# Attention and mixture of experts on one core: the order of the turns in attention, passes of 64 instead of 128 tokens, and a third path

## The chip, the cores and the metric

The kernel runs on one core of one Trainium2 chip. A core has TensorE (matrix products), VectorE, ScalarE and GpSimd (POOL) for the rest, and SyncE, which here only issues DMA transfers. The metric is the device time of one execution in microseconds; the median of three executions is 398.88 us (398.73 to 399.06).

## What is computed

Windowed attention with 8 heads over 4 batches of 576 tokens, then each token goes to one of 8 experts (two layers, ReLU between), and its row is scaled by its gate value:

```python
scores = scale * np.matmul(q, k.transpose(0, 1, 3, 2))
bias = slopes[:, None, None] * (-np.abs(rel).astype(np.float32))[None, :, :]
mask = (rel >= 0) & (rel < window)                    # window = 128
scores = np.where(mask, scores + bias[None], -1000000000.0)
attn = softmax(scores); x = attn @ v                  # x: 2304 rows of 512
logits = x @ w_gate; expert_idx = np.argmax(logits, axis=1)
h = np.maximum(x_e @ w1[e], 0.0)                      # per expert, 512 -> 1024
y = h @ w2[e]; out[i] = gate_w[i] * y                 # 1024 -> 512
```

With the inputs of the reference the eight experts get 373, 244, 350, 293, 183, 193, 328 and 340 tokens. The capacity of 576 drops none.

## The kernel before

**Attention.** Queries are taken in 18 tiles of 128 tokens, in two spans of 9, and each tile in two steps of four heads ("quads"): 18 steps (`kk`) in each of two calls of `batch`. In one step TensorE does, in the order written in `batch` of the tensor block: a turn (four transposes) of the q rows (even steps) or k rows (odd steps) of the tile two ahead into the one PSUM bank `turn_ps`; the transposes of this step's probabilities (`turn_probs`); the turn back of the mix of the step before, with the gate logits (`turn_back`); the scores of the step two ahead (`score`); and the mix of this step (`mix`), first with `v_rows`, then with `v_step`, the difference of two tiles' v. ScalarE copies the mix (`copy_mix`), the turned q (`turned_q`) and the turned probabilities (`turned_probs`), and takes the exponentials of the next step (`exps`). VectorE copies the turned k, replaces masked scores (`pick`), adds the bias and takes minima (`bias_minimum`), and scales the result (`normalise`). GpSimd masks the turned probabilities (`keep_later`, line 624), makes `v_step` (line 605) and, in steps 4 to 19, splits the first expert's weights into a high and a low part (lines 616 and 617). A bank is shared by the scores of a step and the turn back of the step before the last, so `turn_back` waits for `biased`, the minima of the scores that lay there. The routing of the tokens (top expert, ranks, slots) is put between these steps in the second call: `early_counts` at `kk` 4 and 13, a first inversion at `kk` 10, and at `kk` 14 the turn of a first gathered tile of expert 0, whose low part VectorE makes at line 1036.

**Experts.** Every product is three matmuls, of high and low parts. Expert 0's first tile has code of its own (`first_...`). Then follow eight groups, `group(n)`: for `c` in 0 to 9, `step` runs chunk `c` of the first layer (12 matmuls, up to `c` = 7, with the tokens as the moving columns) and chunk `c - 2` of the second layer (3 matmuls of 512 columns for each tile of 128 tokens). One pass is one `c`. Group 0 has two tiles. The others have three where the expert has more than 256 tokens, and else two: a branch on a register (`third`, lines 1512 and 1514) picks one of two blocks of code in each pass. The register is loaded at line 1580 in front of each group. ScalarE takes the ReLU's high part of each chunk (`relu`), VectorE the low part (`lower`), and both split the next expert's weights (`split_hi`, `split_lo`), a piece per chunk. The rows of the next group are gathered by GpSimd and turned by TensorE behind passes 3, 4 and 5 (`turn_rows`, tiles 0 to 2; tiles 0 and 2 use the same PSUM bank). All three tiles are turned, used or not. At the group's end `weigh_all` scales each output tile on VectorE and GpSimd scatters it to `out` (line 694); in the last pass the three tiles end one behind the other. `make_tables` computes on VectorE, in group 0 behind `lower` of chunk 0, what the scatter and some rest tiles need.

## Time and profile before

| | |
|---|---|
| median of three executions | 398.88 us |
| the profiled execution | 398.74 us, span 397.0 us |
| mean granted clock of TensorE | 0.993 |
| TensorE busy | 378.6 us, 95% of the span |
| VectorE, ScalarE, GpSimd busy | 252.9, 202.7, 144.4 us |
| attention | up to about 135 us |
| first tile, routing | about 135 to 153 us |
| eight groups | about 153 to 386 us |
| scatter and end | 386 to 397 us |

Times inside the trace are microseconds from the start of the span. A matmul's length in a row is that of its way through the array, and the next one starts before it ends. So what a matmul costs is the distance from one start to the next. Idle time of an engine counts only where somebody waits for it.

### The profile page before, as it was taken

The numbers are of one execution on the slowest core, as the hardware profiler recorded it, in microseconds if no ns is written. First come the engines' busy times: TensorE is split into PE (matmuls) and PEld (weight loads), VectorE is DVE, ScalarE is ACT, GpSimd is POOL, SyncE is SP. The second block draws the span as 40 slices with busy tenths as digits, with TensorE's granted clock in tenths as the row PEclk, the third lists the DMA queues.
The fourth block names the chain that finished last, engine by engine and source line by source line (L and its number), as shares of the span: only waits on it lengthen the run. The fifth ranks groups of instructions, "written<-read, shape, count | busy, mean of one in ns | idle before, by whom it ended". The sixth has DMA issues, their size and how long they took to land.

```text
span 397.0 us, 8382 instructions
## 1 busy us (share of the span) xinstructions
PE 378.6 (95%) x2990; PEld 327.4 (82%) x2990; DVE 252.9 (64%) x796; ACT 202.7 (51%) x535; POOL 144.4 (36%) x192
## 2 busy tenths in 40 slices
PE   7899999998999999999999999999999999999990
PEld 7688777887877778889998989899999899999970
DVE  6787787799898555967665545556768674441120
ACT  2978788886877425536634415434646444411100
POOL 7549989835743432042250121024051340020002
PEclk9999999999999999999999999999999999999997
DMA  9998999999720121887666356354777673010001
GB/s 167 205 305 208 236 225 233 272 260 211 151 85 34 49 45 52 270 260 245 195 226 201 114 181 223 115 187 147 234 254 227 201 223 132 2 54 17 2 2 70
DMA packets 81314, 64.71 MB, mean 163 GB/s; under 512 B 63982, under 2 KB 63982, under 8 KB 81264
## 3 DMA queue, kind: packets, MB, share of 16 engines
q1 hardware_dynamic: 73600, 52.19, 48.2%
q0 software_dynamic: 3840, 11.03, 8.6%
q10 hardware_dynamic: 3824, 0.80, 1.2%
q8 instruction: 34, 0.56, 0.6%
q14 instruction: 16, 0.13, 0.1%
HBM read 54.56 MB, written 11.02 MB: 165 GB/s over the span
## 4 chain that ended last, share of the span: by engine, by line
PE 76%; POOL 10%; DVE 6%; issue 2%; DMA 2%; ACT 1%; SPq 1%; POOLq 0%; DVEq 0%
PE ps L1472 57%; PE ps L1330 4%; POOL weights_sb L617 4%; PE ps L1303 4%; PE ps L1341 3%; PE ps L1465 3%; PE ps L1269 2%; DMA q_rows<-in_q 2%; POOL probsT L624 2%; PE ps L1311 2%; POOL v_step L605 2%; POOL weights_sb L616 2%; DVE ps L905 1%; DVE probs L918 1%; POOL out L694 1%
## 5 line engine op out<-in xcount | busy, mean ns | idle before, releaser
L1472 PE MATMUL ps<-rowsT_hi,weights_sb 128*128 128x256 f32 (+1 forms) x512 | 120.7, 313 | 0.7 <-DVE rowsT_lo L1156 0.7
L1472 PE MATMUL ps<-weights_sb,hiddenT 128*128 128x512 f32 x480 | 118.3, 392 | 0.8 <-DVE hiddenT L1173 0.8
L1472 PEld LDWEIGHTS ps<-weights_sb,hiddenT 128*128 128x128 f32 x480 | 88.1, 188 | 17.3 <-DVE hiddenT L1173 1.0
L855 ACT ACTIVATE hiddenT<-ps 128x384 fp32r<-128x384 f32 (+1 forms) x64 | 30.6, 479 | 117.3 <-PE ps L1472 110.7
L1472 PEld LDWEIGHTS ps<-rowsT_hi,weights_sb 128*128 128x128 f32 x512 | 87.6, 188 | 2.2 <-DVE rowsT_lo L1156 1.1
L1181 DVE TENSOR_TENSOR weights_sb<-raw,weights_sb 128x1024 fp32r<-128x1024 f32 x56 | 68.5, 1223 | 18.1 <-ACT weights_sb L843 15.2
L1472 PE MATMUL ps<-rowsT_lo,weights_sb 128*128 128x256 f32 (+1 forms) x256 | 79.0, 309 | 0.0
L1173 DVE SCALAR_TENSOR_TENSOR hiddenT<-ps,hiddenT 128x384 fp32r<-128x384 f32 (+1 forms) x64 | 34.5, 539 | 62.1 <-ACT hiddenT L855 62.1
L843 ACT ACTIVATE weights_sb<-raw 128x1024 fp32r<-128x1024 f32 x56 | 58.9, 1052 | 0.2 <-DMA raw<-in_moe_w 0.2
L680 POOL DMA_INDIRECT gathered<-x_rows,src_row x21 | 21.7, 1035 | 95.5 <-DVE weight_now L1167 90.9
L694 POOL DMA_INDIRECT out<-y_sb,dst_row x21 | 24.4, 1161 | 86.9 <-DVE y_sb L1187 82.6
L741 ACT ACTIVATE probs<-probs,mins 128x128 f32<-128x128 f32 x144 | 55.6, 393 | 0.4 <-DVE mins L918 0.4
L1472 PEld LDWEIGHTS ps<-rowsT_lo,weights_sb 128*128 128x128 f32 x256 | 48.2, 188 | 1.1
L624 POOL TENSOR_SCALAR_AFFINE_SELECT probsT<-probsT 128x512 f32<-128x512 f32 x32 | 20.4, 638 | 41.6 <-ACT probsT L767 41.6
L1303 PE MATMUL ps<-kT,qT 64*64 64x192 f32 (+3 forms) x480 | 28.8, 332 | 0.0
L741 ACT ACTIVATION_READ_ACCUMULATOR probs<-probs,mins 128x1 f32 x144 | 27.7, 192 | 0.0
L767 ACT ACTIVATE probsT<-ps 128x512 f32<-128x512 f32 x36 | 21.4, 594 | 10.2 <-PE ps L1311 10.2
L1341 PE MATMUL ps<-eye_wg,mixT 128*128 128x144 f32 x144 | 24.2, 291 | 2.5 <-DVE mins L918 2.5
L905 DVE COPY_PREDICATED ps<-later,ps 128x256 f32<-128x256 int32 (+1 forms) x64 | 22.1, 391 | 4.9 <-PE ps L1303 4.7
L947 DVE TENSOR_TENSOR x_sb<-ps,inv_sums 128x256 f32<-128x256 f32 x36 | 15.3, 424 | 15.3 <-PE ps L1341 13.5
L1187 DVE TENSOR_SCALAR y_sb<-ps,weight_now 128x512 f32<-128x512 f32 x23 | 15.9, 745 | 14.2 <-PE ps L1472 14.2
L1330 PE MATMUL ps<-probsT,v_rows 128*64 128x128 f32 x288 | 23.7, 285 | 0.1
(173 smaller groups left out, 494.2 us busy)
## 6 DMA issues: line engine op xcount, KB each, us to landing
raw<-in_moe_w SPq DMA_DIRECT2D x64, 512.0 KB, 4.4
q_rows<-in_q SPq DMA_DIRECT2D x16, 256.0 KB, 5.9
v_rows<-in_v SPq DMA_DIRECT2D x16, 256.0 KB, 5.2
x_rows<-x_sb SPq DMA_DIRECT2D x16, 256.0 KB, 4.5
k_rows<-in_k SPq DMA_DIRECT2D x14, 256.0 KB, 6.3
k_rows<-in_k ACTq DMA_DIRECT2D x2, 256.0 KB, 6.7
v_rows<-in_v SPq DMA_DIRECT2D x4, 128.0 KB, 5.9
v_front<-in_v SPq DMA_DIRECT2D x4, 128.0 KB, 6.4
```

Of the source, the lines that this page charges most:

```text
L624: g.affine_select(out=probsT[:, 1, :, :], in_=probsT[:, 0, :, :], compare_op=ALU.is_gt, fill=0.0, base=0, pattern=[[0, QUAD], [-1, P]], ch ...
L694: g.indirect_dma_start(out, bass.IndirectOffsetOnAxis(ap=rows[:, i:i + 1], axis=0), y_sb[:, i, :], None, bounds_check=N - 1, oob_is_err=Fa ...
L741: last = nc.scalar.activation(pr, pr, ACT.Exp, bias=mins[:, kk % 2, n:n + 1], scale=-1.0, accum_out=sums[:, i, h:h + 1])
L843: nc.scalar.activation(weights_sb[:, parity(e), 2 * layer, RAW * j:RAW * (j + 1)], raw[:, j, :], ACT.Copy).then_inc(w_hi[layer], 1)
L855: nc.scalar.activation(hiddenT[0][c % RINGED][:, 0:P * size], hiddenT_ps(c, size), ACT.Relu).then_inc(hiddenT_hi, 1)
L905: vec.copy_predicated(both[:, :, 2 * P - earlier[i]:2 * P], later[:, own].bitcast(I32).unsqueeze(1).broadcast_to([P, 2, earlier[i]]), both ...
L1173: vec.scalar_tensor_tensor(out=hiddenT[1][c % RINGED][:, 0:P * size], in0=hiddenT_ps(c, size), scalar=0.0, in1=hiddenT[0][c % RINGED][:, 0 ...
L1181: vec.tensor_tensor(weights_sb[:, parity(e), 2 * layer + 1, part], raw[:, j, :], weights_sb[:, parity(e), 2 * layer, part].bitcast(F32), A ...
L1303: ins = te.matmul(scores_ps(kk % 2, odd)[rows, 2 * P * n + first:2 * P * n + last], qT[part, u % 2, h // 2, rows], keys, start=True, stop= ...
L1330: last = te.matmul(mixT_ps[DH * odd:DH * odd + DH, n, :], left[:, DH * h:DH * h + DH], probsT[:, part, 2 * odd + n, :], start=(part == 0), ...
L1341: last = te.matmul(back_ps(kk % 2)[:, c, :], mixT[:, c, :], eye_wg[:, 2 * quad + c, :], start=True, stop=True)
L1472: ins = te.matmul(dst, left[a], right[c], start=first and n == 0, stop=last and n == 2)
```

## The change

In attention the turn of q or k goes behind the transposes of the probabilities (except in the very first step), and ScalarE copies the turned q behind the exponentials. The routing's counts and the first inversion go ahead of `turn_back`. VectorE makes the first tile's low part behind the minima of its step. In the expert layers, tile 1 of group 0 is turned right behind tile 0. `third` has three values: none, half (up to 320 tokens, first-layer passes of 320 columns instead of 384) and whole. A third tile that isn't used isn't turned. The register for the next group is loaded at the start of a group. `make_tables` is cut in two, and its long part goes to group 1. In the last group the last three chunks of the second layer run tile by tile.

```diff
@@ ScalarE, batch
+                    if first and kk == 0:
+                        turned_q(b, 2)
+                    turned_probs(b, kk)
+                    if not (last and kk == STEPS - 1):
+                        exps(b + (kk + 1) // STEPS, (kk + 1) % STEPS)
-                    if quad == 0 and not (last and i + 2 >= TI):
+                    if quad == 0 and not (last and i + 2 >= TI) and not (first and kk == 0):
                         turned_q(b + (i + 2) // TI, (i + 2) % TI)
...
-                    turned_probs(b, kk)
-                    if not (last and kk == STEPS - 1):
-                        exps(b + (kk + 1) // STEPS, (kk + 1) % STEPS)
@@ VectorE
-            vec.tensor_scalar(third_i[:, :], tiles_of[:, :], float(SIDE), None, ALU.is_ge).then_inc(sizes_ready, 1)
+            counts = late_ranks_ps[:, E * FULL:E * FULL + E]
+            link(vec.tensor_scalar(extra[:, :], counts, float(P * (SIDE - 1)), None, ALU.is_gt))
+            vec.scalar_tensor_tensor(out=third_i[:, :], in0=counts, scalar=float(P * (SIDE - 1) + HALF),
+                                     in1=extra[:, :], op0=ALU.is_gt, op1=ALU.add).then_inc(sizes_ready, 1)
...
-                    if n == 0 and c == 0:
+                    if n == 0 and c == 2:
+                        make_targets()
+                    if n == 1 and c == 2:
                         make_tables()
@@ TensorE, batch
-                    if turns and quad == 0:
...
+                    if first and kk == 0:
+                        turn_next()
+                    turn_probs(b, kk, 0)
+                    turn_probs(b, kk, 1)
+                    if not (first and kk == 0):
+                        turn_next()
...
-                    turn_probs(b, kk, 0)
-                    turn_probs(b, kk, 1)
-                    if first and kk == 1:
-                        pe.wait_ge(wg_landed, 48)
-                    if not (first and kk == 0):
-                        turn_back(b + (kk - 1) // STEPS, (kk - 1) % STEPS)
                     if last and kk == FIRST_INVERTED:
...
+                    if not (first and kk == 0):
+                        turn_back(b + (kk - 1) // STEPS, (kk - 1) % STEPS)
@@ TensorE, experts
+            def last_chunks(n, size):
+                for i in range(size):
+                    for c in range(FC - RINGED, FC):
+                        if i == 0:
+                            pe.wait_ge(hiddenT_ready, n * FC + c + 1)
+                        last = product(y_ps(i), [part[c % RINGED][:, P * i:P * i + P] for part in hiddenT],
+                                       [weights(parity(n), kind, D * c, D) for kind in (2, 3)], False, c == FC - 1)
+                    last.then_inc(y_done[i], 1)
...
+            def turn_third(n, third):
+                with pe.If(third > 0):
+                    turn_rows(n, SIDE - 1)
+                with pe.If(third < 1):
+                    pe.wait_ge(rowsT_ready, tile_count(n, 0))
+                    pe.sem_inc(rows_turned[SIDE - 1], 1)
...
             def group(n, third):
+                after = third_of(n + 1) if n + 1 < E else None
                 for c in range(FC + RINGED - 1):
...
-                        with pe.If(third > 0):
+                        with pe.If(third > 1):
                             step(n, SIDE, c)
+                        with pe.If(third < 2):
+                            with pe.If(third > 0):
+                                step(n, SIDE, c, HALF)
                         with pe.If(third < 1):
                             step(n, SIDE - 1, c)
...
             turn_rows(0, 0)
-            first_second_layer(range(FC - 2, FC - 1))
             pe.wait_ge(filled_ready, 1)
             turn_rows(0, 1)
-            first_second_layer(range(FC - 1, FC)).then_inc(first_y_done, 1)
+            first_second_layer(range(FC - 2, FC)).then_inc(first_y_done, 1)
             rows_and_weights(0)
-            group(0, None)
+            pe.wait_ge(sizes_ready, 1)
+            third = group(0, None)
```

The order of TensorE in an odd step of attention (step 1; `probs` are the probabilities, `k_rows` the turn, `mixT` the turn back), before:

```order
L1269 MATMUL ps<-ident,k_rows 128x128 [waits k_landed2,qT_ready]
L1269 MATMUL ps<-ident,k_rows 128x128 x3
L1311 MATMUL ps<-ident,probs 128x128 [waits probs_ready]
L1311 MATMUL ps<-ident,probs 128x128
L1311 MATMUL ps<-ident,probs 128x128 [waits probs_ready]
L1311 MATMUL ps<-ident,probs 128x128
L1341 MATMUL ps<-eye_wg,mixT 128x144 [waits mixT_ready,biased,wg_landed]
```

and after:

```order
L1324 MATMUL ps<-ident,probs 128x128 [waits probs_ready]
L1324 MATMUL ps<-ident,probs 128x128
L1324 MATMUL ps<-ident,probs 128x128 [waits probs_ready]
L1324 MATMUL ps<-ident,probs 128x128
L1282 MATMUL ps<-ident,k_rows 128x128 [waits k_landed2,qT_ready]
L1282 MATMUL ps<-ident,k_rows 128x128 x3
L1354 MATMUL ps<-eye_wg,mixT 128x144 [waits mixT_ready,biased,wg_landed]
```

The two kinds of transposes have changed places; what each waits for is the same.

TensorE from the turn of group 0's first tile (`gathered`) to the first matmul of group 0 (`rowsT_hi`), before:

```order
L1465 MATMUL ps<-ident,gathered 128x128 [waits gather_done0]
L1465 MATMUL ps<-ident,gathered 128x128 x3
L1472 MATMUL ps<-weights_sb,first_hiddenT_hi 128x512 x2
L1472 MATMUL ps<-weights_sb,first_hiddenT_lo 128x512
L1465 MATMUL ps<-ident,gathered 128x128 [waits gather_done1,filled_ready]
L1465 MATMUL ps<-ident,gathered 128x128 x3
L1472 MATMUL ps<-weights_sb,first_hiddenT_hi 128x512 x2
L1472 MATMUL ps<-weights_sb,first_hiddenT_lo 128x512
L1472 MATMUL ps<-rowsT_hi,weights_sb 128x256 [waits w1_split,rowsT_ready]
```

and after:

```order
L1486 MATMUL ps<-ident,gathered 128x128 [waits gather_done1,filled_ready]
L1486 MATMUL ps<-ident,gathered 128x128 x3
L1493 MATMUL ps<-weights_sb,first_hiddenT_hi 128x512 x2
L1493 MATMUL ps<-weights_sb,first_hiddenT_lo 128x512
L1493 MATMUL ps<-weights_sb,first_hiddenT_hi 128x512 x2
L1493 MATMUL ps<-weights_sb,first_hiddenT_lo 128x512
L1550 TENSOR_LOAD third_i [waits sizes_ready,w1_split,rowsT_ready]
L1550 ISA x2
L1493 MATMUL ps<-rowsT_hi,weights_sb 128x256
```

The second turn stands three matmuls earlier, and the load of the register now stands behind the wait for the turned rows and ahead of the first matmul.

## Rows read from the trace of the kernel before

**Rows 1.** Waits of TensorE, whole run: us in total, times, longest.
```profile
PE ps L1341 <- DVE mins L918: 2.5, 3, 1.1
...
PE ps L1472 <- DVE hiddenT L1173: 0.8, 1, 0.8
PE ps L1472 <- DVE rowsT_lo L1156: 0.7, 1, 0.7
```
**Rows 2.** Timeline, attention: start us, length us, engine, line; in brackets idle, releaser.
```profile
31.46 0.33 PE L1269 MATMUL ps<-ident,q_rows 128*128 128x128 f32 x1
...
48.77 1.28 POOL L617 TENSOR_TENSOR weights_sb<-raw,weights_sb 128x512 fp32r<-128x512 f32 x1
...
50.66 0.64 POOL L624 TENSOR_SCALAR_AFFINE_SELECT probsT<-probsT 128x512 f32<-128x512 f32 x1 [0.61 <-ACT probsT L767]
...
69.61 0.33 PE L1269 MATMUL ps<-ident,k_rows 128*128 128x128 f32 x1
...
78.62 0.33 PE L1269 MATMUL ps<-ident,q_rows 128*128 128x128 f32 x1
...
81.97 0.33 PE L1269 MATMUL ps<-ident,k_rows 128*128 128x128 f32 x1
```
**Rows 3.** Timeline, attention: first steps, counts of the routing, first tile's low part.
```profile
15.07 0.20 PEld L1311 LDWEIGHTS ps<-ident,probs 128*128 128x128 f32 x2 [0.20 <-ACT probs L741]
...
86.94 0.20 PE L1352 MATMUL ps<-onehot,below 128*128 128x72 bf16 x1
...
87.58 0.72 PE L1303 MATMUL ps<-kT,qT 64*64 64x192 f32 x12
...
125.04 0.69 DVE L1036 TENSOR_TENSOR first_rowsT_lo<-ps,first_rowsT_hi 128x512 fp32r<-128x512 f32 x1
```
**Rows 4.** Timeline of TensorE in the expert layers, passes of 256 and 384 tokens.
```profile
172.29 0.28 PE L1472 MATMUL ps<-rowsT_lo,weights_sb 128*128 128x256 f32 x1
...
173.59 0.63 PE L1472 MATMUL ps<-weights_sb,hiddenT 128*128 128x512 f32 x2
...
214.84 0.51 PE L1472 MATMUL ps<-rowsT_hi,weights_sb 128*128 128x384 f32 x2
...
216.57 2.25 PE L1472 MATMUL ps<-weights_sb,hiddenT 128*128 128x512 f32 x9
...
218.66 0.60 PE L1465 MATMUL ps<-ident,gathered 128*128 128x128 f32 x4
...
219.28 0.34 PE L1472 MATMUL ps<-rowsT_lo,weights_sb 128*128 128x384 f32 x1
```
**Rows 5.** Timeline of VectorE before expert 0's group, and line 1580: ns, first and last start.
```profile
151.00 0.69 DVE L1156 TENSOR_TENSOR rowsT_lo<-ps,rowsT_hi 128x512 fp32r<-128x512 f32 x1 [2.81 <-ACT rowsT_hi L848]
...
152.13 0.69 DVE L1156 TENSOR_TENSOR rowsT_lo<-ps,rowsT_hi 128x512 fp32r<-128x512 f32 x1 [0.43 <-ACT rowsT_hi L848]
...
L1580 PEldq TENSOR_LOAD <-third_i x7: 301/312/483, 174.8 to 349.1; - x7
...
L1580 PEldq SEQ_ASSERT  x7: 18/18/28, 175.6 to 349.8; - x7
```
**Rows 6.** Timeline of VectorE in group 0, and line 1514 as in rows 5.
```profile
155.35 0.30 DVE L1218 SCALAR_TENSOR_TENSOR is_free<-is_free,src_f 128x144 f32<-128x144 f32 x1
...
159.31 0.17 DVE L1241 TENSOR_SCALAR column_i<-column_f 128x18 int32<-128x18 f32 x1
...
L1514 PEldq COMPARE_BRANCH  x70: 72/210/353, 176.2 to 382.1; - x70
```
**Rows 7.** DMA queues of the page: packets, MB, share of 16 engines.
```profile
q8 instruction: 34, 0.56, 0.6%
```
**Rows 8.** Timeline of the end.
```profile
385.18 2.07 DVE L1187 TENSOR_SCALAR y_sb<-ps,weight_now 128x512 f32<-128x512 f32 x3 [3.87 <-PE ps L1472]
386.72 0.98 POOL L694 DMA_INDIRECT out<-y_sb,dst_row  x1 [29.80 <-DVE y_sb L1187]
...
389.30 0.99 POOL L694 DMA_INDIRECT out<-y_sb,dst_row  x1 [0.30 <-issue]
```

More of the change, by code:

```diff
@@ L337, in attention_moe @@
         is_full_ready = sem("is_full_ready")
-        rows_turned = sem("rows_turned")
+        rows_turned = [sem(f"rows_turned{i}") for i in range(SIDE)]
         rowsT_hi = sem("rowsT_hi")
@@ L669, in gather @@
                 if not (isinstance(n, int) and n == 0):
-                    pool.wait_ge(rows_turned, tiles_before(n))
+                    for i in range(sides(n)):
+                        if not (isinstance(n, int) and n == 1 and i == SIDE - 1):
+                            pool.wait_ge(rows_turned[i], n if i < SIDE - 1 else n - 1)
                     pool.wait_ge(weight_kept, n)
@@ L1057, in batch @@
                             bias_minimum(b + (kk + 2) // STEPS, (kk + 2) % STEPS, odd)
+                    if last and kk == STEPS - 4:
+                        dve.wait_ge(first_rows_hi, 1)
+                        vec.tensor_tensor(first_rowsT[1][:, :, :], turn_ps.rearrange("p (c s) -> p c s", c=DC),
+                                          first_rowsT[0][:, :, :].bitcast(F32), ALU.subtract
+                                          ).then_inc(first_rows_ready, 1)
                     if last and since == 1:
@@ L1220, in make_tables @@
                 vec.tensor_copy(dst_row[:, :], is_free[:, :]).then_inc(dst_ready, 1)
+            def make_tables():
                 te = [P, TABLE, E]
@@ L1428, in batch @@
                         n = 0 if kk == 4 else 1
+                        pe.wait_ge(mixT_ready, b * STEPS + kk)
                         pe.wait_ge(onehot_ready, n + 1)
                         early_counts(n).then_inc(ranked, 1)
+                    if first and kk == 1:
+                        pe.wait_ge(wg_landed, 48)
+                    if not (first and kk == 0):
+                        turn_back(b + (kk - 1) // STEPS, (kk - 1) % STEPS)
                     if not (last and kk + 2 >= STEPS):
@@ L1476, in weights, with first_layer @@
                 return weights_sb[:, slot, kind, at:at + size]
-            def first_layer(n, size, c):
+            def first_layer(n, tokens, c):
                 for d in range(DC):
-                    last = product(hiddenT_ps(c, size), [weights(parity(n), kind, F * d + P * c, P) for kind in (0, 1)],
-                                   [part[:, d, 0:P * size] for part in rowsT[parity(n)]], d == 0, d == DC - 1)
+                    last = product(hiddenT_ps(c, tokens), [weights(parity(n), kind, F * d + P * c, P) for kind in (0, 1)],
+                                   [part[:, d, 0:tokens] for part in rowsT[parity(n)]], d == 0, d == DC - 1)
                 last.then_inc(hidden_done, 1)
@@ L1494, in second_layer, with step @@
                         last.then_inc(y_done[i], 1)
-            def step(n, size, c):
-                if c < FC:
-                    first_layer(n, size, c)
-                if c >= RINGED - 1:
+            def last_chunks(n, size):
[6 more added lines that the diff above has]
+                    last.then_inc(y_done[i], 1)
+            def step(n, size, c, spared=0):
+                if c < FC:
+                    first_layer(n, P * size - spared, c)
+                by_tiles = isinstance(n, int) and n == E - 1
+                if by_tiles and c == FC + RINGED - 2:
+                    last_chunks(n, size)
+                elif RINGED - 1 <= c < (FC - 1 if by_tiles else FC + RINGED - 1):
                     second_layer(n, size, c - (RINGED - 1))
@@ L1517, in group @@
                                 pe.sem_inc(y_done[SIDE - 1], 1)
-                    if c in TURNED_AT and n + 1 < E:
+                    if c in TURNED_AT[:-1] and n + 1 < E:
                         turn_rows(n + 1, c - TURNED_AT[0])
+                    if c == TURNED_AT[-1] and n + 1 < E:
+                        turn_third(n + 1, after)
+                return after
             def first_tile_chunks(half, chunks):
```

39 lines of the change are left out of this document (19 added, 20 removed).

## Prediction

> **What bounds the kernel now.** I read the waits of TensorE first. TensorE is busy 95% of the span, and of the little that it waits, three pieces lie behind the start: 2.5 us in three waits of the turn back for VectorE's minima, 0.8 us in group 0 for the low part of a hidden chunk, and 0.7 us in front of group 0 for the low part of the turned rows [rows 1]. All else must be sought in the distances between its starts. In attention an undisturbed step of TensorE lasts 3.35 us (from the turn at 78.62 to that at 81.97), but the eleven steps from 31.46 to 69.61 last 38.15 us and not 36.85 [rows 2]. GpSimd splits weights there, and the rows show why it holds the others up though it isn't full: its subtraction ends at 48.77 + 1.28 = 50.05, then it sits idle for 0.61 us until ScalarE has copied the turned probabilities, and masks them at 50.66 [rows 2]. In the groups TensorE runs without a gap but one, and everything else has slack. So the expert part gets shorter only by less work on TensorE, by closing those two waits, or by a shorter tail behind its last matmul.
>
> **The sum is made against the profiled execution's 398.74 us,** 0.14 below the median. The 1.74 us outside the span stay.
>
> **Attention, GpSimd's stretch: -1.3.** The turn no longer stands ahead of the probabilities. A turn of four transposes costs about 0.45 us (from 218.66 to 219.28 is one turn and one matmul of 0.173, below) [rows 4]. So ScalarE's copy and GpSimd's mask can start about 0.45 us earlier in the step. GpSimd's work in a pair of steps is the pair's length less the idle 0.61, and the pair lasts about 2 x 38.15 / 11 = 6.94: that is 6.3 us, less than TensorE's 2 x 3.35 = 6.70. TensorE becomes the bound, and the excess of 38.15 - 36.85 = 1.3 goes. The bounds are 0 (something else holds the steps at their length) and -1.5. The q that ScalarE now copies last is wanted by the next step's k turn, which itself stands later; I give that nothing. It would cost at most what ScalarE lacks in one step, and it has idle time in every step there.
>
> **Attention, first steps: +0.3.** In step 1 the exponentials aren't ready: TensorE turned k and still waited 0.20 us for them, until 15.07 [rows 3]. With the turn behind, it has nothing to fill with, and the whole turn of 0.45 to 0.5 comes after. What was hidden is now in the open, less the time for which the first half of the probabilities can go ahead. Bounds 0 and 0.5.
>
> **Attention, counts ahead of the turn back: +0.65.** The 14 small matmuls of the counts last 87.58 - 86.94 = 0.64 us [rows 3]. They stood behind `turn_back`, where they held up only the scores. Now they hold up the turn back too, and behind it VectorE's `normalise`, which stands ahead of the next `pick`. It is from these three places (`kk` 4, 10 and 13) that VectorE's long stretches start at whose ends TensorE waits the 2.5 us [rows 1]. VectorE has some slack before each, so not all of 0.64 arrives. I take 0.25, 0.3 and 0.1. Bounds 0 and 1.6 (three times the 0.64, less one smaller group).
>
> **Attention, low part of the first tile: -0.6.** Its 0.69 us at 125.04 [rows 3] stood in VectorE's queue ahead of the minima for which TensorE waits at the third place, one of the three waits of [rows 1]. Behind them it is wanted only ten microseconds later. The minima come 0.69 earlier less the 0.1 above, and that wait is about as long. Bounds 0 and -0.7. Attention in all: -0.95.
>
> **In front of group 0: +0.2.** Here two edits pull against each other. With tile 1 turned right behind tile 0, ScalarE and VectorE can run back to back: the first low part lasts from 151.00 to 151.69, and the second can then end at about 152.3 instead of 152.13 + 0.69 = 152.82 [rows 5], if the gathered rows have landed by then. That alone would take 0.5 of the 0.7 us wait. But the register's load now stands behind that very wait and ahead of the first matmul, where TensorE's queue is empty. A load and what belongs to it takes from 174.8 to 175.6 in its first instance, and 0.7 in its last [rows 5]. Between the groups this is hidden, because the sequencer runs ahead of the array: the trace has no gap at 174.8. Here it has nothing to hide behind. -0.5 + 0.7 = +0.2. Bounds -0.5 (hidden after all) and +0.4.
>
> **The hole in group 0: -0.8.** `make_tables` holds VectorE from 155.35 to 159.48 [rows 6], and the low part of chunk 1 comes 0.8 us too late for TensorE [rows 1]. The short part that stays (two of the operations) stands behind chunk 2, when that chunk is done. The long part, about 3.3 us, goes to group 1 behind chunk 2. Who waits there is the low part of chunk 3, which TensorE wants two passes later, and two passes of a two-tile group last 2 x 2.8 us (12 x 0.118 + 6 x 0.232, both below). VectorE has the split of one piece (1.2) to do besides, so about 1 us of slack remains. Bounds -0.9 and 0.
>
> **Turns of unused third tiles: -1.2.** Experts 1, 4 and 5 have 256 tokens or fewer. Three turns at 0.36 to 0.45 [rows 4], all on a TensorE that doesn't wait. ScalarE and VectorE still copy.
>
> **Half passes: -2.65.** Only expert 3, with 293 tokens, is between 257 and 320. The distance between matmuls of 256 columns is (173.59 - 172.29) / 11 = 0.118 us, with 384 it is (216.57 - 214.84) / 10 = 0.173 [rows 4]. A straight line gives 0.0275 less for 320 than for 384, times 8 x 12 = 96 matmuls: 2.65 us. The second layer has the tokens as weights and doesn't change. Its distance of 0.232 ((218.66 - 216.57) / 9) stays [rows 4]. Nothing near the 0.118 of the narrower pass can stop a distance of 0.146, so both loading and streaming allow it. Bounds -2.65 and 0.
>
> **More branches: 0.** In each of the 70 passes one more comparison, or two, is executed. One that jumps took 0.21 us, one that falls through 0.07 [rows 6]. So the sequencer needs some 0.3 us more for each pass, and a pass lasts at least 1.4. The cover is the sequencer's lead, which hid 0.7 to 0.8 us of loading between groups.
>
> **The end: -1.25.** Output tiles used to end 3 matmuls apart, now they end 9 apart (2.1 us). The last one ends when it did, and VectorE's scaling with it, at 385.18 + 2.07 = 387.25. But the scatters were queued on GpSimd: the first started at 386.72, 0.8 after its tile's scaling, and the third only at 389.30 [rows 8]. Now the two before it are long gone, and it starts at 387.25 + 0.8 = 388.05. 1.25 earlier; what follows it is the same. The wait for the last hidden chunk has only 6 matmuls of cover (1.4 us) instead of 18; the ReLU and low part take about that, so I give 0 and at worst 0.2.
>
> **Sum:** -0.95 + 0.2 - 0.8 - 1.2 - 2.65 - 1.25 = -6.65, so 392.1 us.
>
> **Rivals.** *VectorE or ScalarE takes GpSimd's place in attention.* The steps keep their length, or the three stretches of VectorE grow by all of 0.64 each. For it speaks that VectorE's stretches start from places that come later now; against it, that between 30 and 80 us VectorE has idle time in each step. It gives 0 to +1.5 for attention instead of -0.95: 393.0 to 394.5, say 393.6.
>
> *The half passes don't pay, or aren't taken* (the distance stays at 0.173, or the register says 2 for expert 3). Nothing in the trace has 320 columns. 392.1 + 2.65 = 394.7.
>
> *More goes than I count* (the load hidden, the counts harmless): 392.1 - 0.7 - 0.65 = 390.7.
>
> *Code loading makes it slower.* Each pass now holds three blocks of code. By the order of instructions a group of the seven has 492 matmuls instead of 324, each with its load of weights, so the program grows by 7 x 168 x 2 = 2,350 instructions, from about 9,200. The 34 packets of the instruction queue carried 0.56 MB [rows 7]: the growth is some 9 packets more. A packet took 0.006 x 16 x 397 / 34 = 1.1 us. If each is in the open, TensorE stands for 9 x 1.1 = 10 us, and the time is 402; it decides from 0.75 us for each. Against it: the 34 of now leave no gap in the groups. Advanced Engine Details and Errata (ISA Cache) in the Trainium skill says that a line of the instruction cache holds 16 KB or 256 instructions, which agrees with 0.56 MB in 34 packets.
>
> **How the numbers follow.** 0.64 for my sum, 0.2 for the steps of attention that don't gain, 0.06 for the half passes that don't pay, 0.06 for more, 0.04 for code loading. The range of 390.4 to 394.7 takes in the first four. A measurement of this kernel can tell about 0.2% (0.8 us) from no change. All cases but the last lie clearly below 398.1: faster 0.95, same 0.01, slower 0.04.
>
> **What would show it.** Turns 3.35 us apart between 31 and 70 us. A wait of the turn back after the counts that has grown at the first two places and nearly gone at the third. No wait for hiddenT in group 0, and a gap of about 0.9 us in front of group 0 with the register's load in it. 96 matmuls of 320 columns in one group, 0.145 apart, and 80 transposes of gathered rows instead of 92. The last scatter about 1.3 us closer to TensorE's last matmul. I am wrong if TensorE shows gaps at the passes' starts, if the low part of chunk 3 of group 1 is waited for, or if attention ends no earlier.

## Result: 1.0% faster, and attention longer instead of shorter

| | before | changed |
|---|---|---|
| median | 398.97 us (398.73 to 399.41, 4 runs) | 395.06 us (393.71 to 395.72, 4 runs) |
| the profiled execution | 398.74 us, span 397.0 | 393.71 us, span 391.9 |
| mean granted clock in the profile | 0.993 | 0.994 |

The ratio is 0.990 (95% interval 0.988 to 0.992). The direction was right and the size wrong: 392.1 was forecast, and the median lies 0.4 us above the range. Two things need an explanation: the profiled execution is 1.6 us slower than the sum, and it is the fastest of four, whose times spread over 2.0 us.

I cut the trace where the first tile's first matmul starts, where group 0 starts, and at the last matmul's start:

| stretch, us | before | changed | difference | forecast |
|---|---|---|---|---|
| up to the first tile (attention) | 135.58 | 136.45 | +0.87 | -0.95 |
| first tile, to the start of group 0 | 17.30 | 17.58 | +0.3 | +0.2 |
| eight groups, to the last matmul's start | 233.13 | 228.16 | -4.97 | -4.65 |
| from there to the end of the span | 11.02 | 9.71 | -1.31 | -1.25 |

So the expert part did what the sum said, and attention alone failed, by 1.8 us. The arrival of the first q and k differs from run to run: the first mix starts at 13.32 instead of 13.64 here, so counted from there attention grew by 1.2. I number attention's steps from 0 to 35 (the second span begins with 18) and measure each from the start of the last mix of the step before to that of its own.

| step | before | changed | what is new |
|---|---|---|---|
| 1 | 3.31 | 3.58 | the turn is in the open |
| 6 to 15, each | 3.40 to 3.52 | 3.35 | GpSimd no longer holds them up |
| 16 | 3.51 | 3.19 | the same |
| 20 | 3.40 | 4.21 | the turn back waits 0.54 |
| 22 | 4.09 | 4.38 | counts ahead of the turn back |
| 24 | 4.80 | 5.36 | the turn back waits 1.29 instead of 1.11 |
| 28 | 3.67 | 3.97 | inversion ahead of the turn back |
| 30 | 4.29 | 4.04 | |
| 31 | 3.98 | 4.23 | counts ahead of the turn back |
| 33 | 3.86 | 3.65 | the low part no longer in the way |
| 34 | 2.68 | 3.35 | the turn back waits 0.98 |

GpSimd's stretch gained what it should. In the timeline of TensorE, eleven steps after the probabilities' transposes at 31.41 come those at 68.11: 36.70 us, against 38.15 between the turns of [rows 2].

```profile
31.41 0.66 PE L1324 MATMUL ps<-ident,probs 128*128 128x128 f32 x4
...
68.11 0.66 PE L1324 MATMUL ps<-ident,probs 128*128 128x128 f32 x4
```

The waits of TensorE, changed kernel (us in total, times, longest), answer to [rows 1]. The turn back waits longer and oftener, the wait for `hiddenT` in group 0 is gone, and small ones are new, two of them of the mix. The counts and the inversion write to a bank that the mix uses too, and VectorE reads them only behind `normalise`, which waits for the turn back. Before, the counts stood between the turn back and the mix and gave VectorE that time. Now they stand ahead of both, and the mix waits.

```profile
PE ps L1354 <- DVE mins L922: 3.7, 5, 1.3
...
PE ps L1493 <- DVE rowsT_lo L1163: 1.0, 1, 1.0
...
PE ps L1343 <- DVE own_rank L996: 0.3, 1, 0.3
PE ps L1343 <- DVE first_slot L1049: 0.2, 1, 0.2
```

**What the minima waited for.** I looked at what GpSimd (POOL) and VectorE (DVE) do ahead of the three long waits, at steps 20, 24 and 34. The columns are start, length, engine, line, and in brackets the idle time with its releaser.

```profile
75.81 1.27 POOL L617 TENSOR_TENSOR weights_sb<-raw,weights_sb 128x512 fp32r<-128x512 f32 x1
75.96 1.15 DVE L938 TENSOR_TENSOR sums_eps<-sums,eps 128x8 f32<-128x8 f32 x1
78.77 0.51 PE L1354 MATMUL ps<-eye_wg,mixT 128*128 128x144 f32 x2 [0.54 <-DVE mins L922]
...
90.38 0.63 POOL L624 TENSOR_SCALAR_AFFINE_SELECT probsT<-probsT 128x512 f32<-128x512 f32 x1 [3.74 <-ACT probsT L769]
90.40 0.64 DVE L1015 TENSOR_SCALAR past<-rounded 128x9 f32<-128x9 f32 x1
90.98 1.28 POOL L605 TENSOR_TENSOR v_step<-v_rows 128x512 f32<-128x512 f32 x1
91.08 1.21 DVE L1016 SCALAR_TENSOR_TENSOR key<-best,past 128x9 f32<-128x9 f32 x1
95.21 0.76 PE L1354 MATMUL ps<-eye_wg,mixT 128*128 128x144 f32 x4 [1.29 <-DVE mins L922]
...
128.13 0.69 DVE L1059 TENSOR_TENSOR first_rowsT_lo<-ps,first_rowsT_hi 128x512 fp32r<-128x512 f32 x1
...
128.69 1.27 POOL L605 TENSOR_TENSOR v_step<-v_rows 128x512 f32<-128x512 f32 x1
128.80 1.22 DVE L1025 TENSOR_SCALAR in_tile<-iota_p,within,mark 128x128 f16<-128x128 f16 x1
...
132.01 0.76 PE L1354 MATMUL ps<-eye_wg,mixT 128*128 128x144 f32 x4 [0.98 <-DVE mins L922]
```

An addition of 8 numbers in each row lasts 1.15 us. Each of these VectorE operations starts just behind one of GpSimd's, and ends 0.03 to 0.06 us behind it: 77.11 and 77.08, 91.04 and 91.01, 92.29 and 92.26, 130.02 and 129.96. Where no GpSimd operation runs beside them in the same trace, they last 0.16, 0.17, 0.16 and 0.31 us. The kernel before has two of these places too, but there it is a shorter GpSimd operation that they meet. At step 1, where it meets a `v_step`, the addition lasts 1.13 us even there:

```profile
15.54 1.13 DVE L934 TENSOR_TENSOR sums_eps<-sums,eps 128x8 f32<-128x8 f32 x1
...
77.10 0.58 DVE L934 TENSOR_TENSOR sums_eps<-sums,eps 128x8 f32<-128x8 f32 x1
...
91.27 0.59 DVE L1012 SCALAR_TENSOR_TENSOR key<-best,past 128x9 f32<-128x9 f32 x1
```

The Trainium skill, SBUF — State Buffer, SBUF: two separate sides, says that VectorE and GpSimd share a pair of ports, which the one that starts first holds for its whole instruction while the other is fully blocked. By the same section VectorE needs the pair in a mode that takes both ports, or with two SBUF inputs while GpSimd's instruction reads SBUF. The trace agrees: `sums_eps` and `key`, with two SBUF inputs, are held, and `x_sb`, which reads one operand from PSUM, lasts 424 to 426 ns in all its 36 instances, among them twelve that lie wholly within a GpSimd subtraction. `past` and `in_tile` have one SBUF input and are held too. In which mode they run, no trace shows.

**The expert part.** In front of group 0 TensorE waits 1.01 us instead of the 0.71 that the kernel before shows as 0.7 in [rows 1]. The low part of the rows was ready by 151.86 + 1.29 = 153.15. The register's load, of which the first row gives the first and last start behind the lengths in ns, and what belongs to it are over only at 153.9.

```profile
L1550 PEldq TENSOR_LOAD <-third_i x7: 301/308/484, 153.2 to 312.0; - x7
...
L1550 PEldq SEQ_ASSERT  x7: 18/18/28, 153.9 to 312.5; - x7
```

The timeline of VectorE and TensorE there:

```profile
151.86 1.29 DVE L1163 TENSOR_TENSOR rowsT_lo<-ps,rowsT_hi 128x512 fp32r<-128x512 f32 x2 [2.82 <-ACT rowsT_hi L852]
...
152.62 0.40 PE L1493 MATMUL ps<-weights_sb,first_hiddenT_lo 128*128 128x512 f32 x1
154.03 0.38 PE L1493 MATMUL ps<-rowsT_hi,weights_sb 128*128 128x256 f32 x1 [1.01 <-DVE rowsT_lo L1163]
```

In the groups, by shape (count | busy us, mean ns): 96 matmuls of 320 columns, and 80 transposes instead of 92.

```profile
L1493 PE MATMUL ps<-rowsT_hi,weights_sb 128*128 128x320 f32 x64 | 15.3, 312 | 0.0
L1486 PE MATMUL ps<-ident,gathered 128*128 128x128 f32 x80 | 11.8, 272 | 0.0
L1493 PE MATMUL ps<-rowsT_lo,weights_sb 128*128 128x320 f32 x32 | 9.9, 310 | 0.0
```

In TensorE's timeline six distances between starts lie from 247.58 to 248.46, 0.147 us each. A straight line had given 0.1455.

```profile
247.58 0.31 PE L1493 MATMUL ps<-rowsT_lo,weights_sb 128*128 128x320 f32 x1
...
248.46 0.31 PE L1493 MATMUL ps<-rowsT_lo,weights_sb 128*128 128x320 f32 x1
```

Split at the turns' starts, the -4.97 is -1.07 up to the first turn in group 0 (the hole), -1.36 for the three unused tiles and -2.62 for expert 3's group; under 0.1 is left. The queue of instructions, on the page, answers to [rows 7]: ten packets more, and no start in the groups is over 0.1 us late.

```profile
q8 instruction: 44, 0.72, 0.8%
```

At the end the last scatter is issued at 384.16, 1.97 us after the last matmul's start. In [rows 8] it is issued at 389.30, 3.29 us after.

```profile
380.10 0.98 POOL L696 DMA_INDIRECT out<-y_sb,dst_row  x1 [27.09 <-DVE y_sb L1196]
382.09 0.98 POOL L696 DMA_INDIRECT out<-y_sb,dst_row  x1 [1.00 <-DVE y_sb L1196]
384.16 0.98 POOL L696 DMA_INDIRECT out<-y_sb,dst_row  x1 [1.09 <-DVE y_sb L1196]
```

### The profile page after: what moved, and what is told of

Its sections match the earlier page's. It is cut to its first block, busy times and chain, and to the rows that moved or that the text cites. A ratio compares the mean times of both kernels' runs of the same rounds, so it can differ in the third digit from the quotient of the medians.

```text
span 391.9 us, 8491 instructions
## 1 busy us (share of the span) xinstructions
PE 373.1 (95%) x2978; PEld 323.0 (82%) x2978; DVE 253.9 (65%) x797; ACT 202.3 (52%) x535; POOL 144.6 (37%) x192
## 3 DMA queue, kind: packets, MB, share of 16 engines
HBM read 54.56 MB, written 11.02 MB: 167 GB/s over the span
## 4 chain that ended last, share of the span: by engine, by line
PE 86%; DVE 7%; DMA 2%; ACT 1%; issue 1%; SPq 1%; POOL 0%; DVEq 0%; POOLq 0%
PE ps L1493 59%; PE ps L1343 7%; PE ps L1316 5%; PE ps L1354 4%; PE ps L1324 4%; PE ps L1282 3%; PE ps L1486 2%; DMA q_rows<-in_q 2%; DVE ps L909 1%; DVE probs L922 1%; DVE x_sb L951 1%; DVE kT L932 1%; PE ps L1400 0%; SPq L444 0%; PE ps L1360 0%
## 5 line engine op out<-in xcount | busy, mean ns | idle before, releaser
L1493 PE MATMUL ps<-rowsT_hi,weights_sb 128*128 128x256 f32 (+2 forms) x512 | 118.2, 309 | 1.0 <-DVE rowsT_lo L1163 1.0
L1493 PE MATMUL ps<-rowsT_lo,weights_sb 128*128 128x256 f32 (+2 forms) x256 | 78.2, 306 | 0.0
L1324 PE MATMUL ps<-ident,probs 128*128 128x128 f32 x144 | 23.8, 287 | 0.3 <-ACT probs L743 0.3
```

Source lines behind the costliest of these rows:

```text
L1324: last = te.transpose(probsT_ps[:, P * (2 * odd + n):P * (2 * odd + n) + P], probs[:, kk % 2, 2 * odd + n, :], ident[:, :])
L1493: ins = te.matmul(dst, left[a], right[c], start=first and n == 0, stop=last and n == 2)
```

## Experiments

Two theories stood against each other for attention. H1: VectorE's short operations meet GpSimd's long ones at other places now, and are held for longer. H2: counts and inversion ahead of the turn back cost all of it. The kernel before had medians of 398.96, 398.93, 399.26 and 398.98 us beside the four sets of runs.

**The changed kernel again, and the old order of attention**

> The changed kernel once more, nothing edited. Its first four times ran from 393.71 to 395.72 us, and the lowest goes with the highest mean granted clock (0.994 against 0.990). Theory S (the spread is TensorE's clock falling once or twice behind an idle stretch, most likely the 1.0 us in front of group 0): the times fall again between 393.5 and 396, with the mean clock, and a profile of a slower one shows a slice at 1.2 GHz that the first profile doesn't have. Rival: nothing but the chip's DMA differs: the times spread without the clock.

Measured: 394.87 us median (393.66 to 396.85, 6 runs), ratio 0.990 (0.987 to 0.993). The times spread as forecast, but not for the reason forecast. The mean clock is between 0.987 and 0.994 and follows the time only in part: the slowest run, 396.85, has the lowest, but the fastest, 393.66, has 0.991, and one of 395.21, the profiled one, has 0.993. In that profile step 20 lasts 3.40 us: GpSimd waited 0.84 us for rows of v ahead of it, so its subtraction began only at 77.27, behind the addition at 76.54. Step 24 lasts 5.34, and step 28 5.19 instead of 3.97:

```profile
111.29 0.42 DVE L951 TENSOR_TENSOR x_sb<-ps,inv_sums 128x256 f32<-128x256 f32 x1 [2.52 <-PE ps L1354]
...
112.24 0.66 PE L1343 MATMUL ps<-probsT,v_rows 128*64 128x128 f32 x8 [1.45 <-DVE first_slot L1049]
```

The profile models the turn back named in the first row to end by 109.97, but its signal stands in the trace at 111.20, 1.2 us later. In the first profile it came 0.02 us behind the modelled end. It is this signal that `x_sb` waited for. `normalise` waits for stored rows (`rows_stored`) only ahead of a tile's first quad, and this is the second. Behind `x_sb` stand `first_slot` and the mix, so a whole step moves. Why the signal came late isn't shown.

> The changed kernel with the order of attention of the kernel before (ScalarE's batch, the first tile's low part on VectorE, the turn ahead of the probabilities, counts and inversion behind the turn back), everything else as changed. The traces put first matmul of the first tile at 135.58 us before and 136.45 after. Theory A (attention's reordering lost 0.9 us net, all the gain is in the experts): 0.9 less than the changed kernel, ratio to it 0.998, and against before -5.9 us. Rival B (the prediction's own step, attention gains 0.95): 0.9 more than the changed kernel. If the granted clock also falls less often here, more than 0.9.

```diff
-                    turn_probs(b, kk, 0)
-                    turn_probs(b, kk, 1)
-                    if not (first and kk == 0):
-                        turn_next()
+                    if turns and quad == 0:
+                        if not (first and kk == 0):
+                            pe.wait_ge(kT_ready, tb * TI + ti)
+                        turn_q(tb, ti)
+                    if turns and quad == 1:
+                        pe.wait_ge(qT_ready, tb * TI + ti + 1)
+                        turn_k(tb, ti)
...
+                    turn_probs(b, kk, 0)
+                    turn_probs(b, kk, 1)
+                    if first and kk == 1:
+                        pe.wait_ge(wg_landed, 48)
+                    if not (first and kk == 0):
+                        turn_back(b + (kk - 1) // STEPS, (kk - 1) % STEPS)
                     if last and kk == FIRST_INVERTED:
...
```

ScalarE's and VectorE's batches are put back too. Measured: 393.56 us (393.14 to 393.93, 5 runs), ratio 0.986 (0.984 to 0.988). It is 1.3 us faster than the changed kernel on the same chip, and its times spread over 0.8 us instead of 3.2. Theory A holds by the medians. The trace of this run doesn't show the loss: attention ends at 136.38, 0.07 ahead of the changed kernel's. There too a signal came late: that of the scores stands at 111.29, 1.4 us behind their modelled end, and steps 29 and 30 last 4.14 and 4.66 us instead of the 3.35 and 4.29 of the kernel before.

**GpSimd waits**

> The changed kernel in which GpSimd waits, in the second span alone, with three of its instructions until VectorE is past its short operations (sums_eps; the keys): the split's last subtraction, the mask of step 5 of that span, and each v_step. Nothing is left out. Theory H1 (steps 20, 24 and 34 are long since VectorE's short SBUF operation is held for as long as a GpSimd tensor-tensor of 1.28 us runs): sums_eps at step 19 lasts 0.15 to 0.6 and not 1.15, key at step 24 0.17 and not 1.21, past 0.17 and not 0.64, in_tile at step 33 0.31 and not 1.22; the waits of the turn back, 0.54, 1.29 and 0.98 us, shrink to nothing, 0.1 and 0.1, and attention ends 2.0 to 2.6 us earlier. Theory H2 (counts and inversion ahead of the turn back make these waits): attention ends at most 0.3 us earlier, or later, since GpSimd now starts later.

```diff
                 link(g.tensor_copy(hi, src))
+                if piece == 4 * CHUNKS - 1:
+                    pool.wait_ge(sum_step, 2 * TI + 1)
                 ins = g.tensor_tensor(weights_sb[:, 0, 2 * layer + 1, own], src, hi.bitcast(F32), ALU.subtract)
...
+                    if b == 1 and kk == 5:
+                        pool.wait_ge(keys_ready, 1)
                     if kk >= 2:
                         keep_later(b, kk)
...
+                        if b == 1 and kk >= 3:
+                            pool.wait_ge(sum_step, 2 * u + 1)
                         step_v(u + 1)
```

Measured: 391.73 us (391.39 to 391.93, 5 runs), ratio 0.982 (0.980 to 0.983). Nothing but waits was added, and it is 3.1 us faster than the changed kernel. In its timeline the same operations are short, and GpSimd's start behind them:

```profile
76.20 0.15 DVE L944 TENSOR_TENSOR sums_eps<-sums,eps 128x8 f32<-128x8 f32 x1
76.50 1.28 POOL L619 TENSOR_TENSOR weights_sb<-raw,weights_sb 128x512 fp32r<-128x512 f32 x1 [0.54 <-DVE sums_eps L944]
...
90.00 0.17 DVE L1021 TENSOR_SCALAR past<-rounded 128x9 f32<-128x9 f32 x1
90.20 0.17 DVE L1022 SCALAR_TENSOR_TENSOR key<-best,past 128x9 f32<-128x9 f32 x1
90.58 0.63 POOL L626 TENSOR_SCALAR_AFFINE_SELECT probsT<-probsT 128x512 f32<-128x512 f32 x1 [4.34 <-DVEq L1025]
...
93.29 0.76 PE L1360 MATMUL ps<-eye_wg,mixT 128*128 128x144 f32 x4 [0.23 <-DVE mins L928]
```

Step 20 is 3.40 us, step 24 3.84 and step 34 2.73. Attention ends at 133.97 instead of 136.45, 2.48 us earlier: within the 2.0 to 2.6 of H1, far from the 0.3 of H2. The first mix starts at 13.63 here and not 13.32, so counted from there it is 2.8. The waits were 0.54, 1.29 and 0.98; at step 24 0.23 is left. The times spread over 0.5 us, but the kernels below, with the same waits and one thing more changed, spread over 0.35 to 2.0. So it isn't shown that the waits end the spread.

> The order of attention of the kernel before, the changed experts, and GpSimd's waits. It tells what the reordering alone is worth where no collision blurs it. Theory R (without collisions the reordering does what the prediction summed: -1.3 in GpSimd's stretch and -0.3 around it, +0.3 in the first steps, +0.65 to 0.85 for the counts, -0.5 for the low part): about 0.65 slower than the kernel with the waits and the new order, 392.4 us, its GpSimd stretch (steps 6 to 16) 3.45 us for a step again, and step 24 at about 3.9 instead of 4.80. Rival (the waits alone bring the whole gain and the order none): the same time as with the new order, 391.7 within 0.2.

The edit is the same three waits in the kernel with the old order. Measured: 392.49 us (391.92 to 392.92, 4 runs), ratio 0.984 (0.982 to 0.986). Theory R holds with 0.76 us for its 0.65. This run answers what the reordering is worth. Where the collisions are taken out of both orders, the new one is 0.8 us faster, near the 0.95 of the prediction. Where they are left in, it is 1.3 slower. The waits bring the old order 1.1 us and the new one 3.1.

**Counts and inversion behind the turn back**

> The kernel with GpSimd's waits (391.73 us), in which the counts and the inversion of the first group stand behind turn_back again, as in the kernel before. Theory H2 (they cost what the turn back now waits for them, the prediction's step): steps 22, 28 and 31, 4.38, 3.97 and 4.23 us in the kernel with the waits, fall to 4.09, 3.67 and 3.98 as in the kernel before, and the time by 0.6 to 0.85, to about 391.0. Rival (VectorE's long stretches after them end later by as much): the turn back waits longer at steps 24, 30 and 33, and the time stays within 0.2 of 391.73.

```diff
+                    if not (first and kk == 0):
+                        turn_back(b + (kk - 1) // STEPS, (kk - 1) % STEPS)
                     if last and kk == FIRST_INVERTED:

                         lo, hi = GROUPS[0]
-                        pe.wait_ge(mixT_ready, b * STEPS + kk)
...
-                    if not (first and kk == 0):
-                        turn_back(b + (kk - 1) // STEPS, (kk - 1) % STEPS)
```

Measured: 391.35 us (390.49 to 391.97, 4 runs), ratio 0.981 (0.979 to 0.982). Between the two theories: steps 22, 28 and 31 fall by 0.14, 0.18 and 0.18 only, and steps 23 and 24 grow by 0.20 and 0.08. From step 21 to 35 the two traces differ by 0.24 us, the medians by 0.38. H2 exists, but it is the smaller part, and a difference of 0.4 is at the edge of what these runs tell apart.

**The expert part's terms, on the kernel with the waits**

> The kernel with GpSimd's waits, in which the register says a whole third tile wherever there is one, so no pass runs with half of it (expert 3 has 293 tokens). Prediction's step: 96 matmuls back from 0.1465 to 0.173 us, +2.55, to 394.3 us. Rival (a part of the half pass's gain is lost to its branches): less than 2.55, down to 2.0.

```diff
-            vec.scalar_tensor_tensor(out=third_i[:, :], in0=counts, scalar=float(P * (SIDE - 1) + HALF),
+            vec.scalar_tensor_tensor(out=third_i[:, :], in0=counts, scalar=float(P * (SIDE - 1)),
```

Measured: 394.11 us (393.88 to 394.23, 4 runs), ratio 0.988 (0.987 to 0.990): +2.38. In the trace expert 3's group takes 2.6 us longer. The half passes' term stands.

> The kernel with GpSimd's waits, with the last group's second layer chunk by chunk to the end as in the kernel before, so the three output tiles end 3 matmuls apart. Prediction's step: the scatters queue again, last matmul to end of the span 11.0 us instead of 9.7, +1.25 to +1.3 us, to 393.0 us. Rival (the end is set by the last tile's own scatter, and the two ahead of it hide): +0.3 or less.

```diff
-                by_tiles = isinstance(n, int) and n == E - 1
+                by_tiles = False
```

Measured: 392.72 us (392.55 to 393.77, 4 runs), ratio 0.986 (0.984 to 0.987): +1.0. From the last matmul's start to the end it takes 11.00 us instead of 9.69, but the groups took 0.3 less in this trace. GpSimd's three scatters queue with 0.3 us between them, as in [rows 8]:

```profile
380.26 0.98 POOL L702 DMA_INDIRECT out<-y_sb,dst_row  x1 [29.80 <-DVE y_sb L1202]
381.55 0.98 POOL L702 DMA_INDIRECT out<-y_sb,dst_row  x1 [0.31 <-issue]
```

> The kernel with GpSimd's waits, in which VectorE computes the targets and the tables again behind chunk 0 of group 0, as in the kernel before. Prediction's step: TensorE waits 0.8 us for the low part of chunk 1 in group 0 again, 391.73 + 0.8 = 392.5. Rival (group 0 now starts as late after the first tile's end as the front's load makes it, and VectorE is ahead by that): 0.4 or less.

```diff
-                    if n == 0 and c == 2:
+                    if n == 0 and c == 0:
                         make_targets()
-                    if n == 1 and c == 2:
                         make_tables()
```

Measured: 392.39 us (392.3 to 393.16, 4 runs), ratio 0.983 (0.981 to 0.984): +0.66. Against the kernel before beside each (398.96 and 399.26) it is only +0.36, so the medians don't tell the 0.8 from the rival's 0.4. The trace does: the eight groups take 228.90 us instead of 228.15. The hole is back, 0.54 us of waiting and 0.82 between the starts. It is smaller than the 0.8 of [rows 1]:

```profile
160.44 0.73 PE L1498 MATMUL ps<-weights_sb,hiddenT 128*128 128x512 f32 x2 [0.54 <-DVE hiddenT L1188]
```

**The register's load in front of group 0**

> The changed kernel in which the register with group 1's third tile is loaded behind the first pass of group 0 and not in front of group 0. Theory L (the load of 0.48 us and what belongs to it stands in the open): the idle time in front of group 0 falls from 1.01 to 0.3 to 0.5 us, and the time by 0.5 to 0.7 us; and if this idle time is what lets the clock fall (theory S), the times spread less and lie nearer to 393. Rival (the wait for the low part ends last anyway): 1.01 stays within 0.1, since rows_lo is ready only then.

```diff
-                after = third_of(n + 1) if n + 1 < E else None
+                after = third_of(n + 1) if 0 < n < E - 1 else None
                 for c in range(FC + RINGED - 1):
+                    if n == 0 and c == 1:
+                        pe.wait_ge(sizes_ready, 1)
+                        after = third_of(1)
...
-            pe.wait_ge(sizes_ready, 1)
             third = group(0, None)
```

Measured: 394.40 us (393.8 to 395.81, 6 runs), ratio 0.988 (0.986 to 0.990). The idle time in front of group 0 falls from 1.0 to 0.2 us, so the load did stand in the open. The median is 0.5 below that of the changed kernel beside it, less than either spread. In the trace 0.4 comes back at once. Group 0 reaches its first turn of group 1's rows earlier than their gather does. A spread of 2.0 us stays without this idle time, so theory S falls. TensorE's start of group 0 in its timeline:

```profile
155.23 0.38 PE L1493 MATMUL ps<-rowsT_hi,weights_sb 128*128 128x256 f32 x1 [0.19 <-DVE rowsT_lo L1163]
```

and the new wait (us in total, times, longest):

```profile
PE ps L1486 <- DMA gathered<-x_rows,src_row: 0.2, 1, 0.2
```

This profile also shows the clock's part in the spread. Step 24 lasts 6.63 us and step 25 3.65, 1.57 more than in the first profile for both. The table by stretches has the granted clock behind the five busy times:

```profile
94.00:95.50 1.50, 0.37 (x4) 0.13 (x2) 1.50 (x7) 0.12 (x1) 1.50 (x4) 1.00 0.75 217
95.50:96.50 1.00, 0.84 (x4) 0.59 (x4) 0.97 (x8) 0.86 (x5) 0.60 (x1) 0.80 0.97 262
96.50:98.00 1.50, 1.50 (x17) 0.80 (x16) 0.79 (x3) 1.26 (x6) 0.00 (x0) 0.50 1.20 246
98.00:99.50 1.50, 1.50 (x18) 1.50 (x16) 1.37 (x9) 0.00 (x0) 0.00 (x0) 0.50 0.97 248
99.50:101.00 1.50, 1.50 (x17) 1.33 (x14) 0.80 (x7) 0.95 (x3) 0.00 (x0) 1.00 0.38 90
```

Behind two waits close together, 0.23 us and the 1.29 us of step 24, TensorE runs about 3 us at 1.2 GHz instead of 2.4. The first profile has the same two waits at the same place and the full clock. So this idle time doesn't bring the drop about each time, and that it does so at all isn't shown. In no profile of a kernel with the waits is step 24 that long.

> The kernel with GpSimd's waits (391.73 us), and the register load of group 1 behind the first pass of group 0. In the run with the load alone moved, the wait in front of group 0 fell from 1.0 to 0.2 us, and 0.4 came back at the first turn of group 1, which then waited for its gathered rows. Theory: 0.4 us less here too, 391.3. Rival (with attention 2.5 us shorter GpSimd issues the gathers earlier, so nothing comes back): 0.8 less, 390.9.

Measured: 391.53 us (391.09 to 393.1, 4 runs), ratio 0.981 (0.979 to 0.984). The trace agrees with the 0.4 (from the first turn of group 0's rows to the last matmul 231.16 us instead of 231.59). The median moved by 0.2, or 0.5 against the kernel before beside each, which these runs can't tell from nothing. Its times spread over 2.0 us.

> The same, and the counts and the inversion behind turn_back as before: all that the runs so far found to be in the way. If the gains add up: 391.35 less 0.4, 390.9 to 391.0, and ratio to the kernel before 0.980. Rival (they share a wait): 391.3.

Measured: 391.56 us (390.95 to 392.31, 5 runs), ratio 0.980 (0.979 to 0.982). That is above both the theory's 391.0 and the rival's 391.3: the gains didn't add up. Its profiled execution, 392.31, is the slowest of the five, and shows why. These are GpSimd, VectorE and TensorE at steps 19 and 20:

```profile
77.42 1.28 POOL L605 TENSOR_TENSOR v_step<-v_front,v_rows 128x512 f32<-128x512 f32 x1 [1.56 <-DMA v_rows<-in_v]
...
79.33 1.27 POOL L619 TENSOR_TENSOR weights_sb<-raw,weights_sb 128x512 fp32r<-128x512 f32 x1
79.37 1.32 DVE L988 SCALAR_TENSOR_TENSOR code<-is_top,iota_eE 128x72 f32<-128x72 f32 x1
80.55 0.64 POOL L626 TENSOR_SCALAR_AFFINE_SELECT probsT<-probsT 128x512 f32<-128x512 f32 x1
81.33 0.66 PE L1349 MATMUL ps<-probsT,v_step 128*64 128x128 f32 x8 [0.57 <-POOL probsT L626]
```

A piece of the raw weights and then the rows of v landed late, GpSimd's whole queue slid by 3.3 us, the split met another VectorE operation, and the mask behind it came too late.

**The last split moved**

> Counts and inversion behind turn_back, and GpSimd's waits, but the last split of weights moved instead of waited for: it stands two steps later, behind v_step of step 3 of the second span. What is left of the spread came in through this place: in the profile with waits, load and counts together, v_step there started 3.3 us late (it waited 1.56 us for its rows of v), the split ran until 80.60, and the mask behind it came 0.6 us too late for TensorE at step 20. Theory J: step 20 lasts 3.40 us here whenever the rows land, and the times lie between 390.5 and 391.2 with less spread than the 1.5 us of the run with the counts behind, median 391.0. Rival (late rows hold the mask at any rate, and v_step's own late start makes VectorE's operations at step 20 collide): no better than 391.35.

```diff
-                    if 0 <= b * STEPS + kk - 4 < 4 * CHUNKS:
+                    if 0 <= b * STEPS + kk - 4 < 4 * CHUNKS - 1:
                         split_weights(b * STEPS + kk - 4)
+                    if b == 1 and kk == 3:
+                        split_weights(4 * CHUNKS - 1)
```

The base is the kernel with the waits and the counts behind, without the wait in the split. Measured: 391.14 us (390.79 to 391.62, 5 runs), ratio 0.981 (0.979 to 0.982). The spread is 0.8 us, and step 20 3.40, though in this profile the rows landed in time, so J's own case wasn't seen. Three of the five times lie within J's 390.5 to 391.2, the highest doesn't. It has the lowest median of all, 3.9 us below the changed kernel and 7.8 below the kernel before. From the other kernels with the new order and the waits (391.35 to 391.73) it can hardly be told.

## Why the prediction was wrong

**The step that failed** is "Attention in all: -0.95". The profiled execution has +0.87, the medians 1.3 us more than the old order. Point by point:

- *GpSimd's stretch, -1.3*: right. The step's length of 3.35 came, and from the last mix of step 5 to that of step 19 it takes 45.67 us instead of 47.12.
- *First steps, +0.3*: right, +0.27 in step 1.
- *Counts ahead of the turn back, +0.65*: steps 22, 28 and 31 have +0.84 together, but putting the counts back gives 0.24 in the traces and 0.38 in the medians. About half of the term would have been right. It left out one path, the bank shared with the mix.
- *Low part of the first tile, -0.6*: too large. The wait at step 33 fell by 0.2 only. In its new place the low part (128.13 in the timeline above) stands ahead of `in_tile`, which so starts at 128.80, 0.11 behind GpSimd's `v_step`.
- *What was not in the sum at all*: +0.81, +0.56 and +0.67 at steps 20, 24 and 34, 2.0 us. Taking the collisions away gives 2.48 in the traces and 3.1 in the medians. I had treated every duration of VectorE as its own. The trace of before had the clue: operations of 0.16 us that lasted 1.13, 0.58 and 0.59, the last of them ahead of the longest wait in [rows 1]. I read the waits' names, not the durations of the operations ahead of them.

The first rival, "VectorE or ScalarE takes GpSimd's place in attention", was nearest in size (393.0 to 394.5), but by another mechanism: VectorE doesn't get more to do, it is held. Without the collisions the sum of attention's terms is close to the truth: 0.95 forecast, 0.76 measured. That is in part luck, since the counts and the low part were each off by 0.3 to 0.4 and the two errors cancel.

**The expert part was right, term by term:** +0.3 for +0.2 in front of group 0 (the load in the open is confirmed by moving it), -1.07 for -0.8 in the hole (+0.75 in the trace when undone), -1.36 for -1.2 for the unused turns (in the trace only, not undone by itself), -2.62 for -2.65 for the half passes (+2.38 when undone), 0 for the branches, and -1.31 for -1.25 at the end (+1.0 when undone). Together -6.0 for -5.7. Code loading, the slower rival, did nothing.

**The range was too narrow for another reason as well.** The changed kernel's ten times lie between 393.66 and 396.85. The range was made from one trace, as if arrivals of transfers and the places of GpSimd's operations were fixed. Three things were seen to differ between its two profiles and that with the load moved: a collision that happens or not (0.81 us at step 20), a late signal of the turn back (1.2 us at step 28, its cause not shown), and the clock after step 24 (1.57 us). How often each comes was not measured. The executions of 395.67 and 395.72 us in the first set have no trace.

## What to carry over

When a change moves work between queues, lay the new places of GpSimd's operations beside VectorE's, and price each pair that may now overlap. A VectorE operation with both inputs in SBUF can last as long as the GpSimd operation that began ahead of it, however small it is. Look in the trace of before for operations whose longest instance is several times their usual one. Here three waits on the engine with slack were worth 3.1 us, and the better order 0.8 once they were in.

## What the hardware showed

- Which forms of VectorE were held by GpSimd and which not: held were an addition of two SBUF tiles (0.16 to 1.15 us), scalar_tensor_tensor on two SBUF tiles (0.16 to 1.21), and also tensor_scalar with one SBUF input, in f32 (0.17 to 0.64) and f16 (0.31 to 1.22). `x_sb`, with one input in PSUM, wasn't, nor was the reciprocal of 8 values from SBUF, at 202 to 204 ns in eleven instances within a subtraction.
- Matmuls of 320 columns are 0.147 us apart, on the line between 0.118 for 256 and 0.173 for 384.
- With 44 packets of instructions instead of 34 and up to four comparisons in a pass instead of two, no matmul in the groups started over 0.1 us late.
